# The last stage turned: z stationary, token weights moving, and x turned by VectorE and DMAs instead of TensorE

## The chip, the cores and the metric

One core of a Trainium2 chip runs the whole kernel. The metric is the device time of one execution in microseconds, the median of several runs. Granted TensorE clock in the profile is a share of full speed.

## What is computed

Three blocks in a row, for 4 batches of 768 tokens with 384 channels. The first is a gated linear recurrence over 8 heads, the second four attention experts of which each token takes two, the third mixes tokens and then channels. The change lies in the third:

```python
def _moe2_ref(x, w_theta, w_tok_r, w_tok_i, w_ch):
    theta = x @ w_theta
    cos_t, sin_t = (np.cos(theta), np.sin(theta))
    zr = x * cos_t
    zi = x * sin_t
    yr = np.einsum('ts,bsd->btd', w_tok_r, zr)
    yi = np.einsum('ts,bsd->btd', w_tok_i, zi)
    y = yr + yi
    u = x + y
    return (u + np.maximum(u @ w_ch, 0.0)).astype(np.float32)
```

## The kernel before

Every engine has its own program, written out by hand in the order in which it runs, and semaphores tie them. Four passes of a first stage (recurrence, then experts) fill OT, the experts' weighted outputs of all batches. Then the last stage runs over the batches b = 0 to 3, and within a batch over six tiles s of 128 tokens:

- experts_out(b, s) on TensorE makes x and theta of tile s in two PSUM banks (6 and 7). ScalarE copies x to x2 (keep_x2, L626). VectorE folds theta into one turn (fold: fold_first L967 and L969, fold_rest L976 and L979). ScalarE makes sine and cosine (waves, L631 to L634). GpSimd multiplies them by x (L524, in batch 0 L502). ScalarE rounds the product to z_h (z_hi, L639), VectorE subtracts the rest into z_l (z_lo, by the helper at L952).
- mix(s, t) on TensorE adds what tile s gives to each of six token tiles t, in PSUM banks 0 to 5: 128 tokens by 384 channels each. A product in split precision is three matmuls (split_mm, L1253 to L1255), and there are two weights, so a mix is six matmuls, with a piece of the token weights wt_h or wt_l stationary and z moving.
- During mixing of the last tile (s = 5) the channels begin: VectorE adds x to the bank (add_x, L1227), TensorE turns the sum u by three 128x128 transposes (turn_u, L1563), ScalarE rounds it to uT_h (L843), VectorE makes uT_l (L952), TensorE multiplies by w_ch (channels, nine matmuls), VectorE adds the positive part to u (add_relu, L1211), and SP sends the tile out (L421).

In the profile's names digits are left out: x is x2, z_h stands beside wt_h whichever is stationary. In a row of TensorE the operand named first is the moving one. In batch 0 GpSimd also makes wt_l (L496) between its products.

The next batch is started inside the present one: experts_out(it + 1, 0) runs ahead of mixing of tile 5, experts_out(it + 1, 1) behind it, and the first mixing matmul of the next batch waits for z_lo(it + 1, 0), which stands on VectorE behind the last add_relu. SP carries all DMAs on one queue.

The order of TensorE around the end of a batch:

```python
                for t in range(NT):
                    mix(NT - 1, t)
                    if t >= 1:
                        turn_u(t - 1)
                    if t >= 2:
                        channels(t - 2)
```

Of the kernel before, what the change touches and what calls it, by code (L numbers as in the profile page):

```python
# [22 lines left out]
P = 128  # L23
# [136 lines left out]

SLOW = 6
# [29 lines left out]
def build(nc, fT, qT, kT, vT, v, wq, wk, wv, w_gate, wo, woT, w_theta, w_tok, w_ch, out):  # L191
    with ExitStack() as ctx:
# [112 lines left out]
        uT_h = sb("uT_h", [P, 2, D], F32R)  # L305
        uT_l = sb("uT_l", [P, 2, D], F32R)
# [44 lines left out]
        mix_done, u_done, ut_done, uth_done, utl_done = sem("mix_done"), sem("u_done"), sem("ut_done"), sem("uth_done"), sem("utl_done")  # L351
        ch_done, y_ready, x2_free = sem("ch_done"), sem("y_ready"), [sem(f"x2_free{n}") for n in range(NT)]
# [14 lines left out]
        def _(sp):  # L367
# [54 lines left out]
            for n in range(NT):  # L422
                sp.wait_ge(x2_free[n], 16 * (B + 1))
# [105 lines left out]
        def _(act):  # L529
# [93 lines left out]
            def keep_x2(b, s):  # L623
                act.wait_ge(wo_done, upto(b, NT, s + 1))
                act.wait_ge(x2_free[s], upto(b, 16, 16))
                nc.scalar.copy(x2[:, s, :], ps(out_banks(b, s)[0])[:, 0:D]).then_inc(x2_copied, 1)  # L626
# [38 lines left out]
            for it in range(B):  # L665
# [65 lines left out]
                for n in [*range(RING_X), *range(FIRST_QK, RING)]:  # L731
                    if n == FIRST_QK:
                        if it > B - 2:
                            for t in range(NT):
                                act.sem_inc(x2_free[t], 16)
# [87 lines left out]
            for it in range(B):  # L823
# [33 lines left out]
        def _(dve):  # L857
# [350 lines left out]
            def add_relu(b, t):  # L1208

                dve.wait_ge(ch_done, upto(b, NT, t + 1))  # L1210
                nc.vector.scalar_tensor_tensor(out=x2[:, t, :], in0=ps(t)[:, 0:D], scalar=0.0, in1=x2[:, t, :],  # L1211
                                               op0=ALU.max, op1=ALU.add).then_inc(y_ready, 1)

            for it in range(B):
                for s in range(NT - 1):
# [8 lines left out]
                def add_x(t):  # L1224

                    dve.wait_ge(mix_done, upto(it, NT, t + 1))
                    nc.vector.tensor_tensor(x2[:, t, :], ps(t)[:, 0:D], x2[:, t, :], ALU.add).then_inc(u_done, 1)  # L1227
# [16 lines left out]
                add_relu(it, NT - 1)  # L1244
# [5 lines left out]
        def _(pe):  # L1250
# [40 lines left out]
            def mix(s, t):  # L1291
                at = slice(t * P, (t + 1) * P)
# [266 lines left out]
            for it in range(B):  # L1559
                def turn_u(t):  # L1560
                    pe.wait_ge(u_done, upto(it, NT, t + 1))
                    for c in range(NC):
                        mm = nc.tensor.transpose(ps(t)[:, c * P:(c + 1) * P], x2[:, t, c * P:(c + 1) * P],  # L1563
                                                 ident[:, :])
                    mm.then_inc(ut_done, 1)

                def channels(t):
                    pe.wait_ge(utl_done, upto(it, NT, t + 1))
                    for c in range(NC):
                        at = slice(c * P, (c + 1) * P)  # L1570
                        mm = split_mm(ps(t)[:, 0:D], uT_h[:, t % 2, at], uT_l[:, t % 2, at], wch_h[:, c, :],
                                      wch_l[:, c, :], c == 0, c == NC - 1)
                    mm.then_inc(ch_done, 1)

                for s in range(0 if it >= 1 else 1, NT - 1):
# [7 lines left out]
                    for t in range(NT):  # L1583
                        mix(s, t)
# [9 lines left out]
                for t in range(NT):  # L1594
                    mix(NT - 1, t)
                    if t >= 1:
                        turn_u(t - 1)
# [40 lines left out]
```

## Time and profile before

| | |
|---|---|
| median of 3 runs | 568.41 us (567.17 to 569.14) |
| profiled execution | 567.73 us, its span 566.0 us |
| TensorE, VectorE, ScalarE, GpSimd busy | 95%, 65%, 53%, 23% of the span |
| TensorE clock granted | 0.999 |

The span runs from the first to the last recorded event; the execution's own time has 1.7 us more around it. Busy time is that of instructions alone, and TensorE's overlap each other.

### The profile page before, as it was taken

Reading aid. Unit: us, or ns where it says so; the run is one execution under the profiler, and the core shown is the slowest. Engines: PE = TensorE matmul, PEld = TensorE weight load, DVE = VectorE, ACT = ScalarE, POOL = GpSimd, SP = SyncE. Lnnn points to the kernel's source line nnn. Section 1 sums busy time; section 2 is a strip of 40 time slices with the busy share of each in tenths; the row PEclk is TensorE's granted clock in tenths of the full one; section 3 lists DMA queues with packets and bytes.
Section 4 is the critical chain, followed back from the end, with each engine's and each line's share of the span. In section 5 each row is a group of like instructions: output and inputs, shape, how many; then the busy total and the mean of one; then the engine's idle time right before and its main releaser. Section 6 shows DMA issues by size and latency. Waiting matters only on the chain.

```text
span 566.0 us, 14104 instructions
## 1 busy us (share of the span) xinstructions
PE 537.9 (95%) x5996; PEld 507.5 (90%) x5996; DVE 370.4 (65%) x672; ACT 298.0 (53%) x599; POOL 132.1 (23%) x88
## 2 busy tenths in 40 slices
PE   0999999999999999999999999999999999999997
PEld 0789888898789997899977899999999999999997
DVE  2987887888888777865867677555236544562434
ACT  5759687665876558633578574224222433133311
POOL 2004055044510035100123357112211212022200
PEclk9999999999999999999999999999999999999999
DMA  8948003062210530004500000010001100020002
GB/s 288 345 132 307 2 29 86 3 238 79 78 31 3 182 128 2 1 3 136 203 1 2 1 1 2 0 57 30 0 1 43 42 1 1 14 71 1 1 1 83
DMA packets 17969, 37.24 MB, mean 66 GB/s; under 512 B 2160, under 2 KB 10608, under 8 KB 17392
## 3 DMA queue, kind: packets, MB, share of 16 engines
q1 hardware_dynamic: 17904, 36.32, 18.5%
q8 instruction: 47, 0.77, 0.6%
q14 instruction: 18, 0.15, 0.1%
HBM read 31.46 MB, written 4.72 MB: 64 GB/s over the span
## 4 chain that ended last, share of the span: by engine, by line
PE 78%; ACT 8%; DVE 7%; issue 2%; DMA 2%; POOL 1%; SPq 1%; DVEq 0%; POOLq 0%
PE bank L1253 18%; PE bank L1254 18%; PE bank L1255 18%; ACT prob L728 5%; PE bank L1400 4%; PE bank L1271 4%; PE bank L1463 4%; PE bank L1352 3%; PE bank L1316 3%; PE bank L1359 2%; PE bank L1339 2%; DMA OT<-w_theta 2%; ACT probT L769 1%; PE bank L1563 1%; DVE gate L875 1%
## 5 line engine op out<-in xcount | busy, mean ns | idle before, releaser
L1253 PE MATMUL bank<-z_h,wt_h 128*128 128x384 f32 x288 | 97.7, 339 | 0.0
L1254 PE MATMUL bank<-z_l,wt_h 128*128 128x384 f32 x288 | 97.4, 338 | 0.0
L1255 PE MATMUL bank<-z_h,wt_l 128*128 128x384 f32 x288 | 96.5, 335 | 0.0
L728 ACT ACTIVATE prob<-bank,nmax 128x384 f32<-128x384 f32 (+5 forms) x96 | 60.2, 637 | 20.7 <-DVE nmax L1121 20.7
L524 POOL TENSOR_TENSOR trig<-trig,x 128x768 f32<-128x768 f32 x18 | 33.5, 1864 | 149.5 <-ACT trig L634 92.6
L1121 DVE TENSOR_REDUCE nmax<-bank 128x1 f32<-128x384 f32 (+5 forms) x96 | 54.9, 616 | 9.9 <-PE bank L1406 5.2
L967 DVE TENSOR_SCALAR turns<-bank 128x384 int32<-128x384 f32 x22 | 12.2, 556 | 74.0 <-PE bank L1255 74.0
L1253 PEld LDWEIGHTS bank<-z_h,wt_h 128*128 128x128 f32 x288 | 54.0, 188 | 0.6 <-issue 0.3
L1254 PEld LDWEIGHTS bank<-z_l,wt_h 128*128 128x128 f32 x288 | 54.1, 188 | 0.0
L1255 PEld LDWEIGHTS bank<-z_h,wt_l 128*128 128x128 f32 x288 | 54.0, 188 | 0.0
L843 ACT CAST uT_h<-bank 128x384 fp32r<-128x384 f32 x24 | 11.5, 478 | 78.5 <-PE bank L1563 78.5
L1463 PE MATMUL bank<-probT,Vm 128*64 128x128 f32 x672 | 42.0, 276 | 0.8 <-DVE probT L1141 0.2
L1463 PEld LDWEIGHTS bank<-probT,Vm 128*64 128x64 f32 x672 | 36.2, 137 | 2.9 <-DVE probT L1141 1.4
L626 ACT COPY x<-bank 128x384 f32<-128x384 f32 x24 | 11.5, 481 | 49.7 <-PE bank L1255 44.5
L1352 PE MATMUL bank<-V,probT 128*64 128x48 f32 x768 | 36.0, 220 | 1.0 <-ACT xn L681 0.7
L1007 DVE TENSOR_TENSOR probT<-bank,keep 128x1024 f32<-128x1024 f32 x24 | 29.3, 1221 | 11.7 <-PE bank L1271 11.6
L1400 PE MATMUL bank<-qk_h 64*128 64x512 f32 (+3 forms) x128 | 26.2, 406 | 7.1 <-ACT prob L728 5.4
L1253 PE MATMUL bank<-xT_h,wqk_h 128*128 128x384 f32 x96 | 32.9, 343 | 0.0
L1352 PEld LDWEIGHTS bank<-V,probT 128*64 128x64 f32 x768 | 31.3, 138 | 1.5 <-issue 1.2
L1254 PE MATMUL bank<-xT_l,wqk_h 128*128 128x384 f32 x96 | 32.4, 338 | 0.0
L1255 PE MATMUL bank<-xT_h,wqk_l 128*128 128x384 f32 x96 | 32.4, 337 | 0.0
L1141 DVE COPY probT<-bank 128x896 f32<-128x896 f32 x24 | 26.0, 1085 | 7.8 <-PE bank L1316 7.8
(177 smaller groups left out, 1397.7 us busy)
## 6 DMA issues: line engine op xcount, KB each, us to landing
V<-v SPq DMA_DIRECT2D x4, 1152.0 KB, 10.9
gate<-fT SPq DMA_DIRECT2D x12, 384.0 KB, 3.2
q<-qT SPq DMA_DIRECT2D x12, 384.0 KB, 5.8
k<-kT SPq DMA_DIRECT2D x12, 384.0 KB, 6.3
wt_raw<-w_tok SPq DMA_DIRECT2D x6, 768.0 KB, 8.4
out<-x SPq DMA_DIRECT2D x24, 192.0 KB, 1.9
gate<-fT SPq DMA_DIRECT2D x3, 512.0 KB, 4.8
q<-qT SPq DMA_DIRECT2D x3, 512.0 KB, 9.9
```

Of the source, the lines that this page charges most:

```text
L524: nc.gpsimd.tensor_tensor(trig[:, s % 2, :, :], trig[:, s % 2, :, :], x2[:, s:s + 1, :].broadcast_to([P, 2, D]), ALU.mult).then_inc(z_made, 1)
L728: nc.scalar.activation(prob[:, m % 2, r, at], bank[r][:, at], ACT.Exp, bias=nmax[:, m, k:k + 1], accum_out=den[:, m // 2, which, e:e + 1]) ...
L1007: nc.vector.tensor_tensor(Am[:, c % 2, :, :], bank[c % 2][:, :].rearrange("p (h t) -> p h t", h=H), keep[:, None, :].broadcast_to([P, H, P ...
L1121: nc.vector.tensor_reduce(nmax[:, m, k:k + 1], bank[r][:, columns_of(m, which)], X, ALU.max, negate=True).then_inc(max_done, 1)
L1141: nc.vector.tensor_copy(probT[:, m % 2, 1, :].rearrange("p (c h q) -> p h c q", h=2, q=64), turned(m, 1)).then_inc(pt_copied[0], 1)
L1253: nc.tensor.matmul(o, a_h, b_h, start=start, stop=False)
L1254: nc.tensor.matmul(o, a_h, b_l, start=False, stop=False)
L1255: return nc.tensor.matmul(o, a_l, b_h, start=False, stop=stop)
L1271: mm = nc.tensor.matmul(bank[c % 2][:, slot(h):slot(h) + P], k[r:r + 64, h // 2, at], q[r:r + 64, h // 2, at], start=True, stop=True)
L1352: mm = nc.tensor.matmul(ps(out_bank(c))[own, h * HD:(h + 1) * HD], Am[:, c % 2, slot(h) // P, own], V[:, c, h * HD:(h + 1) * HD], start=c ...
L1400: mm = nc.tensor.matmul(bank[r][:, lo_:hi_], x[rows, a, queries], y[rows, 2 + a, keys], start=fresh_bank and n == 0, stop=False, skip_grou ...
L1463: mm = nc.tensor.matmul(ps(values_bank(m))[64 * r:64 * r + 64, at], Vm[:, s, e * ED:(e + 1) * ED], probT[:, m % 2, r, n * P:(n + 1) * P], ...
```

## The change

- Mixing gives its output turned. A piece of z (128 tokens by 128 channels) is stationary and 384 tokens of the token weights move, so that a bank v holds 128 channels (chunk c) by 384 tokens (one half). There are six such groups v, two halves of three chunks (group_of).
- Channels then need no transposes: w_ch is stationary, uT moves. turn_u is gone. Channels start when mixing of all groups is over.
- x must be turned instead, to be added. VectorE's block transpose turns each 32x32 block of x2 into xb (turn_blocks), and when all six tiles of a batch are there, SP moves blocks from partitions 32i to partitions 32j by 16 SBUF-to-SBUF DMAs into uT. The first add_x of a batch waits for them (x_turned).
- Tokens stand in another order (the host permutes w_tok's columns and orders the output back), and the output is written turned, 192 KB a group as before.
- x2 is no longer the output buffer: keep_x2 waits for the last batch's products and block transposes instead of for output DMAs. VectorE's and ScalarE's order at the end of a batch is new, and uT_h and uT_l hold all groups.

```diff
@@ sync
-            with sp.Fori(0, B) as it:
-                for t in range(NT):
-                    sp.wait_ge(y_ready, upto(it, NT, t + 1))
-                    sp.dma_start(out[it, t], x2[:, t, :]).then_inc(x2_free[t], 16)
...
+            for it in range(B):
+                sp.wait_ge(blocks_turned, upto(it, NT, NT))
+                if it >= 1:
+                    sp.wait_ge(out_done, it * 16 * NT)
+                for i in range(QUARTERS):
+                    for j in range(QUARTERS):
+                        sp.dma_start(uT[j * Q:(j + 1) * Q, :, i * NT * Q:(i + 1) * NT * Q],
+                                     xb[i * Q:(i + 1) * Q, j, :, :]).then_inc(x_turned, 16)
+                for g in range(NT):
+                    c, tokens = group_of(g)
+                    sp.wait_ge(y_ready, upto(it, NT, g + 1))
+                    sp.dma_start(out[it, g], uT[:, c, tokens]).then_inc(out_done, 16)
@@ scalar
-                for t in range(NT):
-                    act.wait_ge(ut_done, upto(it, NT, t + 1))
-                    if t >= 2:
-                        act.wait_ge(ch_done, upto(it, NT, t - 1))
-                    nc.scalar.copy(uT_h[:, t % 2, :], ps(t)[:, 0:D]).then_inc(uth_done, 1)
+                for v in range(NT):
+                    c, tokens = group_of(v)
+                    act.wait_ge(u_done, upto(it, NT, v + 1))
+                    nc.scalar.copy(uT_h[:, c, tokens], uT[:, c, tokens]).then_inc(uth_done, 1)
                     if it < B - 1:
-                        if t == 0:
+                        if v == 2:
+                            keep_x2(it + 1, 0)
+                        if v == 3:
                             act.wait_ge(zl_done, upto(it, NT, NT))
                             waves(it + 1, 0)
-                        if t == 3:
-                            keep_x2(it + 1, 0)
-                        if t == 5:
+                        if v == 5:
@@ vector
+            def turn_blocks(b, s):
+
+                dve.wait_ge(x2_copied, upto(b, NT, s + 1))
+                if b >= 1:
+                    dve.wait_ge(ch_done, upto(b - 1, NT, NT))
+                nc.vector.transpose(xb[:, :, :, s * Q:(s + 1) * Q].rearrange("p j c t -> p c j t"),
+                                    x2[:, s, :].rearrange("p (c j t) -> p c j t", c=NC, j=QUARTERS)
+                                    ).then_inc(blocks_turned, 1)
...
                     z_lo(it, s + 1)
+                    if s == 0:
+                        turn_blocks(it, 0)
+                        turn_blocks(it, 1)
+                    elif s == 1:
+                        turn_blocks(it, 2)
+                    if 1 <= s < NT - 2:
+                        turn_blocks(it, s + 2)
...
+                    dve.wait_ge(mix_done, upto(it, NT, v + 1))
+                    if v == 0:
+                        dve.wait_ge(x_turned, (it + 1) * 16 * QUARTERS * QUARTERS)
+                    nc.vector.tensor_tensor(uT[:, c, tokens], ps(v)[:, 0:HALF], uT[:, c, tokens], ALU.add).then_inc(u_done, 1)
...
                 add_x(0)
-                if it < B - 1:
-                    fold_rest(it + 1, 0)
-                for t in range(NT):
-                    if t + 1 < NT:
-                        add_x(t + 1)
-                    dve.wait_ge(uth_done, upto(it, NT, t + 1))
-                    lo(uT_l[:, t % 2, :], ps(t)[:, 0:D], uT_h[:, t % 2, :], utl_done)
-                    if t == NT - 1:
-                        if it < B - 1:
-                            fold(it + 1, 1)
-                    if t >= 1:
-                        add_relu(it, t - 1)
-                add_relu(it, NT - 1)
+                for v in range(1, NT):
+                    add_x(v)
+                    u_lo(v - 1)
+                    if v == NC and it < B - 1:
+                        fold_rest(it + 1, 0)
+                u_lo(NT - 1)
+                for v in range(NT):
+                    add_relu(it, v)
+                    if v == NC - 1 and it < B - 1:
+                        fold(it + 1, 1)
                 if it < B - 1:
                     z_lo(it + 1, 0)
@@ tensor
-                    mm = split_mm(ps(t)[:, 0:D], wt_h[:, n * NT + s, at], wt_l[:, n * NT + s, at],
-                                  z_h[:, s, n, :], z_l[:, s, n, :], s == 0 and n == 0, s == NT - 1 and n == 1)
+                    mm = split_mm(ps(v)[:, 0:HALF], z_h[:, s, n, rows], z_l[:, s, n, rows], wt_h[:, n * NT + s, tokens],
+                                  wt_l[:, n * NT + s, tokens], s == 0 and n == 0, s == NT - 1 and n == 1)
...
+                    if v % NC == 0:
+                        pe.wait_ge(utl_done, upto(it, NT, v + NC))
...
-                for t in range(NT):
-                    mix(NT - 1, t)
-                    if t >= 1:
-                        turn_u(t - 1)
-                    if t >= 2:
-                        channels(t - 2)
+                for v in range(NT):
+                    mix(NT - 1, v)
                 if it < B - 1:
                     banks_read(it + 1, 1)
                     experts_out(it + 1, 1)
-                turn_u(NT - 1)
-                channels(NT - 2)
-                channels(NT - 1)
+                for v in range(NT):
+                    channels(v)
```

VectorE at the end of a batch, before. The first rows are the last channel tiles (x<-bank,x is add_x at L1227 and add_relu at L1211), then the fold of the next batch's tile 1, the last two add_relu and z_l of its tile 0:

```order
L1227 TENSOR_TENSOR x<-bank,x 128x384
L952 TENSOR_TENSOR uT_l<-bank,uT_h 128x384
L1211 SCALAR_TENSOR_TENSOR x<-bank,x 128x384
L952 TENSOR_TENSOR uT_l<-bank,uT_h 128x384
L967 TENSOR_SCALAR turns<-bank 128x384
L969 SCALAR_TENSOR_TENSOR r<-turns,bank 128x384
L976 SCALAR_TENSOR_TENSOR r<-turns,r 128x384
L979 TENSOR_SCALAR r<-r 128x384
L1211 SCALAR_TENSOR_TENSOR x<-bank,x 128x384 x2
L952 TENSOR_TENSOR z_l<-trig,z_h 128x768
```

The same place in the changed kernel (L1272 is add_x, L1237 add_relu, L977 the subtraction, L992 to L1004 the fold):

```order
L1272 TENSOR_TENSOR uT<-bank,uT 128x384
L977 TENSOR_TENSOR uT_l<-uT,uT_h 128x384 x2
L1237 SCALAR_TENSOR_TENSOR uT<-bank,uT 128x384 x3
L992 TENSOR_SCALAR turns<-bank 128x384
L994 SCALAR_TENSOR_TENSOR r<-turns,bank 128x384
L1001 SCALAR_TENSOR_TENSOR r<-turns,r 128x384
L1004 TENSOR_SCALAR r<-r 128x384
L1237 SCALAR_TENSOR_TENSOR uT<-bank,uT 128x384 x3
L977 TENSOR_TENSOR z_l<-trig,z_h 128x768
```

The fold moved from behind the last uT_l to behind the third add_relu, and three add_relu stand between it and z_l instead of two.

SP's queue of the last stage in the changed kernel, from the first batch on:

```order
L443 DMA uT<-xb 32x3x192 [waits blocks_turned]
L443 DMA uT<-xb 32x3x192 x15
L448 DMA out<-uT 128x384 [waits y_ready] x6
L443 DMA uT<-xb 32x3x192 [waits out_done,blocks_turned]
L443 DMA uT<-xb 32x3x192 x15
```

Before, only the output DMAs stood there; now 16 block transfers stand ahead of the six outputs of each batch.

## Rows read from the trace of the kernel before

**Rows 1.** The page, busy us by engine (share of the span) and instructions.

```profile
PE 537.9 (95%) x5996; PEld 507.5 (90%) x5996; DVE 370.4 (65%) x672; ACT 298.0 (53%) x599; POOL 132.1 (23%) x88
```

**Rows 2.** Windows: the last stage, its length, then busy us (instructions) by engine.

```profile
core 0: us, PE busy (x) PEld busy (x) DVE busy (x) ACT busy (x) POOL busy (x), PEclk, DMA share, GB/s
320.00:566.00 246.00, 242.92 (x1435) 241.20 (x1432) 121.78 (x189) 81.63 (x147) 55.44 (x29) 1.00 0.06 20
```

**Rows 3.** Instructions grouped by line: busy us, mean ns, then idle time before.

```profile
L1253 PE MATMUL bank<-z_h,wt_h 128*128 128x384 f32 x288 | 97.7, 339 | 0.0
...
L1563 PE MATMUL bank<-ident,x 128*128 128x128 f32 x72 | 11.7, 271 | 0.0
```

**Rows 4.** The chain of waits, batch 3: start us, us, what.

```profile
547.24 0.33 PE bank L1563 x3
```

**Rows 5.** Timeline of TensorE: start us, us, engine, line, operation.

```profile
381.51 0.33 PE L1253 MATMUL bank<-wx_h,OT_h 128*128 128x384 f32 x1
...
383.59 0.36 PE L1253 MATMUL bank<-z_h,wt_h 128*128 128x384 f32 x1
...
423.43 0.33 PE L1253 MATMUL bank<-z_h,wt_h 128*128 128x384 f32 x1
...
424.48 0.34 PE L1253 MATMUL bank<-z_h,wt_h 128*128 128x384 f32 x1
...
445.36 0.39 PE L1253 MATMUL bank<-z_h,wt_h 128*128 128x384 f32 x1
...
507.23 0.37 PE L1253 MATMUL bank<-z_h,wt_h 128*128 128x384 f32 x1
```

**Rows 6.** Timeline of VectorE in batch 3 (in brackets: idle before, what ended it).

```profile
532.66 0.56 DVE L967 TENSOR_SCALAR turns<-bank 128x384 int32<-128x384 f32 x1 [5.38 <-PE bank L1255]
...
534.72 0.95 DVE L952 TENSOR_TENSOR z_l<-trig,z_h 128x768 fp32r<-128x768 f32 x1
...
546.23 0.56 DVE L1227 TENSOR_TENSOR x<-bank,x 128x384 f32<-128x384 f32 x1 [6.11 <-PE bank L1255]
```

**Rows 7.** Timeline of VectorE, TensorE and GpSimd in batch 0.

```profile
330.47 0.56 DVE L967 TENSOR_SCALAR turns<-bank 128x384 int32<-128x384 f32 x1 [1.18 <-PE bank L1255]
...
335.61 2.60 DVE L952 TENSOR_TENSOR z_l<-trig,z_h 128x768 fp32r<-128x768 f32 x1
...
338.58 0.33 PE L1253 MATMUL bank<-z_h,wt_h 128*128 128x384 f32 x1
...
339.89 3.98 POOL L496 TENSOR_TENSOR wt_l<-wt_raw,wt_h 128x768 fp32r<-128x768 f32 x2
...
340.02 2.14 DVE L976 SCALAR_TENSOR_TENSOR r<-turns,r 128x384 f32<-128x384 int32 x1
...
351.62 0.94 DVE L952 TENSOR_TENSOR z_l<-trig,z_h 128x768 fp32r<-128x768 f32 x1
...
362.88 0.55 DVE L1227 TENSOR_TENSOR x<-bank,x 128x384 f32<-128x384 f32 x1
```

**Rows 8.** DMA issues: KB each and us to landing; issue times; landing of identh's DMAs.

```profile
out<-x SPq DMA_DIRECT2D x24, 192.0 KB, 1.9
...
382.29 0.91 SPq L421 DMA_DIRECT2D out<-x  x2
...
L402 SPq DMA_DIRECT2D identh<-identb x4: 536/596/597, 19.5 to 23.2; - x4
...
DMA to landing us min/median/max: 4.3/5.4/6.5
```

**Rows 9.** Timeline of VectorE and GpSimd at the handover from batch 0 to 1.

```profile
381.30 0.36 DVE L979 TENSOR_SCALAR r<-r 128x384 f32<-128x384 f32 x1
...
382.51 0.94 DVE L952 TENSOR_TENSOR z_l<-trig,z_h 128x768 fp32r<-128x768 f32 x1
...
383.22 1.96 POOL L524 TENSOR_TENSOR trig<-trig,x 128x768 f32<-128x768 f32 x1 [8.79 <-ACT trig L634]
```

**Rows 10.** Timeline of TensorE and VectorE at the end of the program.

```profile
562.58 0.34 PE L1255 MATMUL bank<-wch_h,uT_l 128*128 128x384 f32 x1
...
562.96 0.56 DVE L1211 SCALAR_TENSOR_TENSOR x<-bank,x 128x384 f32<-128x384 f32 x1 [1.01 <-PE bank L1255]
```

More of the change, by code:

```diff
@@ L158, in banks_shared, with group_of @@
     return columns_of(m, 1).stop > 512
+QUARTERS = 4
+Q = P // QUARTERS
+def group_of(v):
+    half, c = divmod(v, NC)
+    return c, slice(half * HALF, (half + 1) * HALF)
 SLOW = 6
@@ L304, in build @@
         trig = sb("trig", [P, 2, 2, D])
-        uT_h = sb("uT_h", [P, 2, D], F32R)
-        uT_l = sb("uT_l", [P, 2, D], F32R)
+        uT = sb("uT", [P, NC, T])
+        blocks_ctx = ExitStack()
+        xb = sb("xb", [P, QUARTERS, NC, NT * Q], where=blocks_ctx)
+        blocks_ctx.close()
+        uT_h = sb("uT_h", [P, NC, T], F32R)
+        uT_l = sb("uT_l", [P, NC, T], F32R)
         after_Am = probT[:, :, :, :].rearrange("p b r n -> p (b r n)")[:, 2 * H * P:2 * H * P + 3 * D]
@@ L350, in build @@
         absd, trig_done, z_made, zh_done, zl_done = sem("absd"), sem("trig_done"), sem("z_made"), sem("zh_done"), sem("zl_done")
-        mix_done, u_done, ut_done, uth_done, utl_done = sem("mix_done"), sem("u_done"), sem("ut_done"), sem("uth_done"), sem("utl_done")
-        ch_done, y_ready, x2_free = sem("ch_done"), sem("y_ready"), [sem(f"x2_free{n}") for n in range(NT)]
+        mix_done, u_done, uth_done, utl_done = sem("mix_done"), sem("u_done"), sem("uth_done"), sem("utl_done")
+        ch_done, y_ready, out_done = sem("ch_done"), sem("y_ready"), sem("out_done")
+        blocks_turned, x_turned = sem("blocks_turned"), sem("x_turned")
         W_QK, W_O, W_OTH, W_CH, W_TH, W_OT = 0, 1536, 2304, 3072, 4224, 5376
@@ L1222, in _, with add_x, u_lo @@
                             split_outputs(it + 1)
-                def add_x(t):
-                    dve.wait_ge(mix_done, upto(it, NT, t + 1))
-                    nc.vector.tensor_tensor(x2[:, t, :], ps(t)[:, 0:D], x2[:, t, :], ALU.add).then_inc(u_done, 1)
+                def add_x(v):
+                    c, tokens = group_of(v)
+                    dve.wait_ge(mix_done, upto(it, NT, v + 1))
+                    if v == 0:
+                        dve.wait_ge(x_turned, (it + 1) * 16 * QUARTERS * QUARTERS)
+                    nc.vector.tensor_tensor(uT[:, c, tokens], ps(v)[:, 0:HALF], uT[:, c, tokens], ALU.add).then_inc(u_done, 1)
+                def u_lo(v):
+                    c, tokens = group_of(v)
+                    dve.wait_ge(uth_done, upto(it, NT, v + 1))
+                    lo(uT_l[:, c, tokens], uT[:, c, tokens], uT_h[:, c, tokens], utl_done)
                 if it < B - 1:
@@ L1559, in _, with channels @@
             for it in range(B):
[L1560 to L1572, printed above, removed]
+                def channels(v):
+                    c, tokens = group_of(v)
+                    if v % NC == 0:
+                        pe.wait_ge(utl_done, upto(it, NT, v + NC))
+                    rows = slice(c * P, (c + 1) * P)
+                    for d in range(NC):
+                        mm = split_mm(ps(v)[:, 0:HALF], wch_h[:, d, rows], wch_l[:, d, rows], uT_h[:, d, tokens],
+                                      uT_l[:, d, tokens], d == 0, d == NC - 1)
                     mm.then_inc(ch_done, 1)
@@ L1582, in _ @@
                         pe.wait_ge(tok_lo, 2 * s + 2)
-                    for t in range(NT):
-                        mix(s, t)
+                    for v in range(NT):
+                        mix(s, v)
                 if it < 1:
@@ L1602, in _ @@
                     experts_out(it + 1, 1)
-                turn_u(NT - 1)
-                channels(NT - 2)
-                channels(NT - 1)
+                for v in range(NT):
+                    channels(v)
 def kernel(**inputs):
@@ L1627 @@
         "w_theta": rows(inputs["moe2_w_theta"]),
-        "w_tok": rows(np.concatenate([inputs["moe2_w_tok_r"].T, inputs["moe2_w_tok_i"].T])),
+        "w_tok": rows(np.concatenate([inputs["moe2_w_tok_r"].T, inputs["moe2_w_tok_i"].T])
+                      .reshape(2 * T, NT, QUARTERS, Q).transpose(0, 2, 1, 3).reshape(2 * T, T)),
         "w_ch": rows(inputs["moe2_w_ch"]),
@@ L1631 @@
     arrays = {n: np.ascontiguousarray(a) for n, a in arrays.items()}
-    nc = bacc.Bacc("TRN2", target_bir_lowering=False, num_devices=1)
+    nc = bacc.Bacc("TRN2", target_bir_lowering=False, num_devices=1, dynamic_dma_scratch_size=8192)
     args = [nc.dram_tensor(n, a.shape, F32, kind="ExternalInput").ap() for n, a in arrays.items()]
-    args.append(nc.dram_tensor("out", (B, NT, P, D), F32, kind="ExternalOutput").ap())
+    args.append(nc.dram_tensor("out", (B, NT, P, HALF), F32, kind="ExternalOutput").ap())
     build(nc, *args)
     r = run_bass_kernel_spmd(nc, [arrays], core_ids=[0])
-    return r.results[0]["out"].reshape(B, T, D)
+    y = r.results[0]["out"].reshape(B, 2, NC, P, QUARTERS // 2, NT, Q)
+    return np.ascontiguousarray(y.transpose(0, 5, 1, 4, 6, 2, 3).reshape(B, T, D))
```

21 lines of the change are left out of this document (11 added, 10 removed).

## The prediction, made before the changed kernel ran

> **What bounds the kernel now.** I began with the page: TensorE is busy 95% of the span, VectorE 65%, ScalarE 53% [rows 1]. The windows show where that is tightest: from 320 us to the end, the last stage, TensorE works 242.9 of 246 us at full granted clock, VectorE 121.8 [rows 2]. In this stage work taken off TensorE is time, as long as nobody else becomes late, so the reader should look for two things: what a TensorE item costs in the stream, and how much room the others have. The grouped lines name the items: 864 mixing matmuls (L1253, and L1254 and L1255 with as many) and the 72 transposes of L1563 [rows 3]. Their mean durations overlap each other and are no price. The price is in the chain of waits, where three transposes together stand for 0.33 us [rows 4]. As a check, the first mixing matmuls of batches 1, 2 and 3 start 61.77 and 61.87 us apart; a batch has 216 mixing, 72 output and 54 channel matmuls, 342 at 0.175 us (six of them lie between 423.43 and 424.48 us), some 59.7 us [rows 5]. Six groups of transposes hold the other 2.1 to 2.2 us, 0.36 us each.
>
> **The change, part by part.**
>
> *TensorE.* It loses 24 groups of three transposes: 24 x 0.36 = **8.6 us off**, all of it on the path. The number of matmuls and their 384 moving columns stay, but in mixing and channels what stands still and what moves is exchanged. The matmuls of the experts' outputs, with other operands in these places, go at 0.173 us (twelve from 381.51 to 383.59) against 0.1745 [rows 5], so the exchange of 216 + 54 matmuls in four batches is worth 1080 x 0.0015 = 1.6 us less, or as much more. I take 0, because both sizes stay.
>
> *VectorE, turning x.* 24 block transposes of 128x384 are added, six a batch, each behind a z_l. No row has this operation. Below stands the quiet 128x384 operation of 0.36 us [rows 9], above the 128x768 subtraction of 0.95 us [rows 6]; I take 0.56, as other 128x384 operations here [rows 6]. That is 3.4 us a batch on an engine that works half of this stage [rows 2], and costs nothing unless it makes the fold behind it late. In batches 1 to 3 that fold waits for TensorE anyway (5.38 us, [rows 6]). Batch 0 is the narrow place: GpSimd splits token weights, z_l took 2.60 us instead of 0.95 and ended at 338.21, and mixing of tile 2 began at 338.58 [rows 7]. But the two transposes ahead of it fill the idle 1.18 us before 330.47, and of the two at 338.2 the second ends at 339.3, 0.45 us after the fold began before; that fold's third operation stands still until GpSimd's instruction is over at 341.9 in any case (2.14 us for 0.56, [rows 7]). I take 0.
>
> That stretching the Trainium skill explains (SBUF — State Buffer, the port pair shared by VectorE and GpSimd): an operation with two SBUF inputs waits for a whole GpSimd instruction that started first. The trace agrees, with those 2.60 us [rows 7]. By the same page a transpose with one input would stay out of it; no row here shows that.
>
> *Block transfers.* Each batch adds 16 DMAs on SP's queue, 72 KB each, SBUF to SBUF. They start when the sixth block transpose is done, and all must have landed before VectorE's first addition of x (L1227 before). Batch 0: z_l of tile 4 ends at 352.56, its transpose at 353.1, and the addition began at 362.88 [rows 7]. Batch 3: 534.72 + 0.95 + 0.56 = 536.2 and 546.23 [rows 6]; batches 1 and 2 have twelve matmuls more in between, 2.1 us. A late addition does not stop TensorE at once. Mixing of tile 5 began 1.25 us before the addition (five matmuls and 0.38 us, [rows 5, 10]), call that M. In batches 0 to 2 the outputs of the next batch's tile 1, wanted 36 matmuls after M, wait for keep_x2, which now stands behind the third uT_h: from the landing two additions, a uT_l, an addition, uT_h and the copy, 4 x 0.56 + 1.1 = 3.3 us. So landing may take until M + 3.0, 364.6 in batch 0. In batch 3 the channels want three uT_l at M + 6.3, seven operations behind the landing, 3.9 us: until 547.4. The rooms are **11.5, 13.8, 13.8 and 11.1 us**. The need: two output DMAs were issued in 0.91 us, 0.46 each, and such a 192 KB landed 1.9 us after issue [rows 8]: 15 x 0.46 + 1.9 = **8.8 us**. The upper bound: of eight SBUF-to-SBUF DMAs of 16 KB, some 0.62 us apart (four of them and what lies between start from 19.5 to 23.2 us), the slowest landed in 6.5 us, with long loads ahead of them [rows 8]: 15 x 0.62 + 6.5 = 15.8 us. I stay by 8.8, since SP's queue is empty here, and take **0 us**, with 2.3 us to spare at the narrowest.
>
> *The order at the end of a batch.* Channels start only when mixing is over, groups 0 to 2 after three uT_l and 3 to 5 after six. VectorE needs 1.11 us a group, mixing 1.05, so three are ready at M + 5.7 and wanted at M + 6.3 (batch 3) or M + 8.4; six are ready by M + 11 and wanted 4.7 us after the first three. Free. The handover is not. The fold of the next batch's tile 1 goes out after the third add_relu instead of after the last uT_l. Count from the start of channels: the third add_relu ends at 4.71 + 0.21 + 0.56 = 5.5 us, the fold 2.1 us later [rows 6] at 7.6; GpSimd's product starts 1.56 us after a fold's end (381.66 to 383.22, [rows 9]), at 9.1, and holds its 1.9 us till 11.0. z_l of the next batch's tile 0 is ready at 10.1, behind the last add_relu, and must wait for it; before, z_l began at 382.51, ahead of GpSimd [rows 9]. It ends at 11.0 + 0.9 = 11.9, and mixing, due at 9.4 + 2.1 = 11.5, starts 0.45 us late. Three handovers: **1.3 us on**. The bounds are 0, if z_l gets there first, and 1.9 us each, a whole GpSimd instruction.
>
> *Rest.* The end of the program is as before, a last matmul, add_relu 0.38 us behind its start, one output DMA [rows 10]: 0. keep_x2 waits for things long over instead of for the output's landing, and SP's loop is written out: 0.
>
> Sum: -8.6 + 1.3 = -7.3 us. The profiled execution took 567.73 us (span 566.0), so 560.4; it stands 0.7 us under the median of the three runs, 568.41, for which I say **561.1 us**.
>
> **Rivals.**
>
> *The blocks land late (0.12).* For it: 16 issues in a row on one queue, each on only 32 partitions, and the bound of 15.8 us. Against: 0.46 us an issue. If a batch's transfers take X us, the stalls above all four rooms are 4X - 50.2; at X = 14.4 they eat the gain, and every us more costs 4. At the bound they are 13.0 us, which makes **574.1 us, slower than before**. With X between 11 and 14.4 the time is 561 to 568.
>
> *One landing after another (0.03).* If each landing were paid in full, 16 x 1.9 = 30.4 us a batch, 4 x 30.4 - 50.2 = 71.4 us more: 632 us. Against: the eight small DMAs went out 0.62 us apart and took 4.3 to 6.5 us, so they overlapped [rows 8].
>
> The Trainium skill (DMA: Bandwidth & Descriptors, anatomy of one DMA) gives a fixed cost of about 2.0 us a transfer, mostly completion; the 1.9 us of rows 8 agree, and as an estimate from that page alone 16 in a row would be 32 us a batch. Its page VectorE: DVE Perf Modes (rules for kernel authors) would keep a 128x128 transpose on TensorE where PSUM will do, which speaks against this change.
>
> *VectorE crowded in batch 0 (0.08).* If the block transposes wait for GpSimd as z_l did, some 1.9 us each, their two pairs push folds back by 2.6 and 3.2 us, against 0.4 us of room at tile 2 [rows 7]: 2 to 5 us of stall, 564.5 us.
>
> *The exchange helps, or the handover costs nothing (0.07).* Matmuls at 0.173 us give 559.5 us, no wait for GpSimd 559.8, most of both 558.8.
>
> **How the numbers follow.** The forecast has 0.70, and the time is its: 561.1 us. The range 558.8 to 566.5 us holds it, the last rival, the crowded batch and the mild part of the late blocks; out are the bad part of these and the serial case. Within 0.3% of 568.4, 1.7 us, is about what a measurement of this kernel cannot tell from no change. Faster: 0.70 + 0.07 + 0.07 (crowded, but not fully) + 0.02 = 0.86. Slower: 0.03 + half of 0.12 = 0.09. Same: the 0.05 left.
>
> **What would show it.** Right: no transposes on TensorE after 324 us, batches about 60.1 us apart, transfers landed before the first addition, a z_l of 1.7 us or more at each handover with TensorE idle some 0.4 us there. Wrong: the first addition released by a DMA later than the rooms above, with TensorE idle behind it; block transposes of over 1 us; matmuls of the last stage off 0.175 us.

## The result, and the profile after

The changed kernel takes **560.51 us** (median of 4 runs, 560.09 to 561.22) against 568.20 us for the kernel before (4 runs, 567.17 to 569.14): a ratio of 0.9869, 95% interval 0.9852 to 0.9886. The prediction was 561.1 us, in a range of 558.8 to 566.5. The profiled execution took 560.85 us, its span is 559.1 us, 6.9 us less than before.

The page after, busy line and chain, with the group of mixing matmuls and the two kinds of DMA of the last stage:

```profile
PE 530.0 (95%) x5924; PEld 499.0 (89%) x5924; DVE 384.8 (69%) x696; ACT 298.7 (53%) x599; POOL 131.9 (24%) x88
...
PE 71%; DVE 11%; ACT 7%; SPq 4%; issue 3%; DMA 2%; POOL 0%; DVEq 0%; POOLq 0%
...
L1301 PE MATMUL bank<-wt_h,z_h 128*128 128x384 f32 x288 | 97.3, 338 | 0.4
...
uT<-xb SPq DMA_DIRECT2D x64, 72.0 KB, 2.1
out<-uT SPq DMA_DIRECT2D x24, 192.0 KB, 1.9
```

TensorE still bounds it, and its matmuls last what they did in [rows 3] (338 ns in the mean, 339 before); the 72 transposes are gone. New in the chain is SPq, SP's queue: the block transfers now stand on the path for a stretch. Where that is can be read from the waits between 320 and 560 us (engine, operation and line that waits, who let it go: us in total, times, longest):

```profile
DVE uT L1272 <- DMA uT<-xb: 12.1, 4, 7.9
...
PEld bank L1301 <- DVE z_l L977: 1.4, 3, 0.5
PEld bank L1301 <- ACT x L654: 1.1, 1, 1.1
...
PEld bank L1301 <- DVE uT_l L977: 0.6, 1, 0.6
```

VectorE waits for the transfers in all four batches. TensorE waits in five places: at three handovers for z_l, and once each for keep_x2 (L654) and for uT_l. The first are the term of +1.3 us of the prediction; the other two it had put at 0. Their places, in order of time (start, duration, engine, line, operation; in brackets the idle time ahead of it and who ended it):

```profile
337.33 2.57 POOL L528 TENSOR_TENSOR trig<-trig,x 128x768 f32<-128x768 f32 x1
...
338.11 1.02 DVE L1245 STREAM_TRANSPOSE xb<-x 128x384 f32<-128x384 f32 x2
...
353.02 10.89 SPq L443 DMA_DIRECT2D uT<-xb  x16
...
362.24 0.55 DVE L994 SCALAR_TENSOR_TENSOR r<-turns,bank 128x384 f32<-128x384 int32 x1
365.52 1.02 DVE L1272 TENSOR_TENSOR uT<-bank,uT 128x384 f32<-128x384 f32 x2 [2.73 <-DMA uT<-xb]
...
367.52 0.34 PE L1303 MATMUL bank<-wt_h,z_l 128*128 128x384 f32 x1
368.66 0.44 PE L1301 MATMUL bank<-wx_h,OT_h 128*128 128x384 f32 x1 [0.80 <-ACT x L654]
...
379.88 1.84 POOL L550 TENSOR_TENSOR trig<-trig,x 128x768 f32<-128x768 f32 x1 [6.47 <-ACT trig L662]
...
380.89 1.65 DVE L977 TENSOR_TENSOR z_l<-trig,z_h 128x768 fp32r<-128x768 f32 x1
...
382.59 0.44 PE L1301 MATMUL bank<-wt_h,z_h 128*128 128x384 f32 x1
...
442.43 0.44 PE L1301 MATMUL bank<-wt_h,z_h 128*128 128x384 f32 x1
...
502.24 0.44 PE L1301 MATMUL bank<-wt_h,z_h 128*128 128x384 f32 x1
...
531.16 10.22 SPq L443 DMA_DIRECT2D uT<-xb  x16
...
542.99 1.02 DVE L1272 TENSOR_TENSOR uT<-bank,uT 128x384 f32<-128x384 f32 x2 [7.87 <-DMA uT<-xb]
...
545.98 0.34 PE L1303 MATMUL bank<-wt_h,z_l 128*128 128x384 f32 x1
546.60 0.45 PE L1301 MATMUL bank<-uT_h,wch_h 128*128 128x384 f32 x1 [0.28 <-DVE uT_l L977]
```

**The transfers.** In batch 0 the addition (L1272) begins 12.5 us after the first issue, in batch 3 11.8 us; the prediction had rooms of 11.5 and 11.1 us for it, and so it was 1.0 and 0.7 us late. TensorE's next matmul starts 1.14 and 0.62 us behind the last one, instead of 0.17: 0.97 and 0.45 us are lost. (The brackets say 0.80 and 0.28, since they count from the end of the last matmul; below, a wait of TensorE is counted from start to start, less 0.17, unless it is called idle.) In batches 1 and 2, with 2 us more room, nothing is.

**The handover** from batch 0 to 1 is the rows from 379.88 to 382.59 us. GpSimd's product, released by the fold that now comes early, starts 1.0 us ahead of z_l, which takes 1.65 us instead of 0.95. The first mixing matmuls of batches 1 to 3 are 59.84 and 59.81 us apart, 61.77 and 61.87 before [rows 5].

### The profile page after: what moved, and what is told of

Same layout as the page of the kernel before. It is cut to its first block, busy times and chain, and to the rows that moved or that the text cites. A ratio compares the mean times of both kernels' runs of the same rounds, so it can differ in the third digit from the quotient of the medians.

```text
span 559.1 us, 13960 instructions
## 1 busy us (share of the span) xinstructions
PE 530.0 (95%) x5924; PEld 499.0 (89%) x5924; DVE 384.8 (69%) x696; ACT 298.7 (53%) x599; POOL 131.9 (24%) x88
## 4 chain that ended last, share of the span: by engine, by line
PE 71%; DVE 11%; ACT 7%; SPq 4%; issue 3%; DMA 2%; POOL 0%; DVEq 0%; POOLq 0%
PE bank L1301 16%; PE bank L1303 15%; PE bank L1302 15%; ACT prob L756 5%; PE bank L1512 5%; PE bank L1319 4%; PE bank L1449 4%; PE bank L1401 3%; SPq L443 3%; PE bank L1365 3%; PE bank L1408 2%; PE bank L1388 2%; DMA OT<-w_theta 2%; DVE gate L900 1%; DVE nmax L1146 1%
## 5 line engine op out<-in xcount | busy, mean ns | idle before, releaser
L1301 PE MATMUL bank<-wt_h,z_h 128*128 128x384 f32 x288 | 97.3, 338 | 0.4
L1303 PE MATMUL bank<-wt_h,z_l 128*128 128x384 f32 x288 | 96.7, 336 | 0.0
L1302 PE MATMUL bank<-wt_l,z_h 128*128 128x384 f32 x288 | 96.5, 335 | 0.0
L992 DVE TENSOR_SCALAR turns<-bank 128x384 int32<-128x384 f32 x22 | 12.2, 554 | 64.7 <-PE bank L1303 64.6
L1301 PEld LDWEIGHTS bank<-wt_h,z_h 128*128 128x128 f32 x288 | 54.0, 188 | 1.7 <-DVE z_l L977 1.4
L1303 PEld LDWEIGHTS bank<-wt_h,z_l 128*128 128x128 f32 x288 | 54.1, 188 | 0.0
L1302 PEld LDWEIGHTS bank<-wt_l,z_h 128*128 128x128 f32 x288 | 54.0, 187 | 0.0
L654 ACT COPY x<-bank 128x384 f32<-128x384 f32 x24 | 11.5, 480 | 56.7 <-PE bank L1303 56.7
L868 ACT CAST uT_h<-uT 128x384 fp32r<-128x384 f32 x24 | 11.8, 511 | 44.6 <-DVE uT L1272 44.4
L659 ACT ACTIVATE trig<-r 128x384 f32<-128x384 f32 x22 | 11.6, 527 | 38.9 <-DVE r L1004 38.9
```

The source lines that it names most:

```text
L1301: nc.tensor.matmul(o, a_h, b_h, start=start, stop=False)
L1302: nc.tensor.matmul(o, a_h, b_l, start=False, stop=False)
L1303: return nc.tensor.matmul(o, a_l, b_h, start=False, stop=stop)
```

## The experiments

The first stage is the same in all these kernels, yet the last stage (VectorE's first turn of a tile's angles, L992, L967 before the change) began between 325.58 and 328.12 us in the profiled executions. So I compare, besides the medians, the **length of the last stage**, from that start to the end of the span: 239.7 us before, 232.8 after. Line numbers shift by a few where lines were added.

### The transfers in whole rows

A transfer writes 32 partitions, 3 runs of 768 bytes on each. Here uT is ordered so that it is one run of 2304 bytes. The outputs, read from the same uT, now go out in two runs of 768 bytes a partition instead of one of 1536.

```diff
-        uT = sb("uT", [P, NC, T])
+        uT = sb("uT", [P, QUARTERS, NC, NT * Q])
...
-                        sp.dma_start(uT[j * Q:(j + 1) * Q, :, i * NT * Q:(i + 1) * NT * Q],
+                        sp.dma_start(uT[j * Q:(j + 1) * Q, i, :, :],
...
-                    sp.dma_start(out[it, g], uT[:, c, tokens]).then_inc(out_done, 16)
+                    sp.dma_start(split(out[it, g]), uT_of(g)).then_inc(out_done, 16)
```

> uT is laid out by token quarter first, so that a block transfer writes one run of 2304 bytes in each of 32 partitions (32 runs a DMA instead of 96); everything else stays. In the changed kernel a transfer takes 0.60 us to issue, 0.64 us apart, and the sixteenth lands 11.8 us after the first was issued (15 x 0.64 + 2.1), which leaves TensorE waiting 1.1 us in batch 0 and 0.9 us in batch 3. Theory A (an issue is priced by its runs): 0.45 us or less an issue, 9 us or less in all, both waits gone, 2.0 us less than the changed kernel, 558.5 us. Theory B (an issue between SBUF and SBUF has a fixed price, as the 64-run DMAs of identh at 0.60 us say): 0.60 us again, 560.5 us.

Measured: 560.73 us (560.45 to 563.39), ratio 0.9876 (0.9849 to 0.9902), last stage 232.7 us. The 16 transfers of batch 0, and the addition behind them (its line is now L1279):

```profile
353.02 10.40 SPq L450 DMA_DIRECT2D uT<-xb  x16
...
364.98 1.02 DVE L1279 TENSOR_TENSOR uT<-bank,uT 128x384 f32<-128x384 f32 x2 [2.25 <-DMA uT<-xb]
```

10.40 instead of 10.89 us, and the addition 12.0 us after the first issue instead of 12.5. With a third of the runs the median issue of a transfer went only from 599 to 591 ns (507 to 1523 here, 591 to 1344 without the edit): fewer runs in what it writes do not make it cheap. The last stage is the same within 0.1 us, but not because nothing changed. TensorE's two waits fell from 0.97 and 0.45 us to 0.49 and 0.30, and its last matmul starts 229.1 us into the stage instead of 229.6. Against that, an output in two runs took 0.53 us to issue and 2.3 us to land, instead of 0.33 and 1.9, so that the time from the last add_relu to the end of the span grew from 2.3 to 2.7 us. The form of a transfer does enter the price of its issue; by what rule, this run does not show.

### The transfers on two queues

Ten stay on SP's queue and six go out from ScalarE.

```diff
+BLOCKS = [(i, j) for i in range(QUARTERS) for j in range(QUARTERS)]
+ON_SP = 10
...
-                for i in range(QUARTERS):
-                    for j in range(QUARTERS):
+                for i, j in BLOCKS[:ON_SP]:
...
+                act.wait_ge(blocks_turned, upto(it, NT, NT))
+                if it >= 1:
+                    act.wait_ge(out_done, it * 16 * NT)
+                for i, j in BLOCKS[ON_SP:]:
+                    act.dma_start(uT[j * Q:(j + 1) * Q, :, i * NT * Q:(i + 1) * NT * Q],
+                                  xb[i * Q:(i + 1) * Q, j, :, :]).then_inc(x_turned, 16)
```

> Six of the sixteen block transfers of a batch are issued by ScalarE, behind its last z_hi, ten stay with SP. If late landing costs the changed kernel 2.0 us (1.1 in batch 0, 0.9 in batch 3): in batch 0 SP's ten land at 353.0 + 9 x 0.64 + 2.1 = 360.9 and ScalarE's six by 361.5, ahead of the first addition; both waits are gone, 558.5 us. If the transfers themselves share something scarce and two queues only interleave, the landing stays at 12 us and the time at 560.5 us. If ScalarE's issues delay its own work more than that, over 560.5.

Measured: 560.0 us (559.23 to 561.38), ratio 0.9858 (0.9832 to 0.9885), last stage 231.3 us. Batch 0:

```profile
353.09 7.19 SPq L446 DMA_DIRECT2D uT<-xb  x10
...
355.22 4.10 ACTq L872 DMA_DIRECT2D uT<-xb  x6
...
362.75 0.55 DVE L1281 TENSOR_TENSOR uT<-bank,uT 128x384 f32<-128x384 f32 x1
```

The addition follows the fold without a wait, and of TensorE's waits in the last stage only the three for z_l are left. The last stage is 1.5 us shorter, about as much as the two waits that are gone (0.97 + 0.45). The late transfers cost 1.5 us. The median is only 0.5 us lower, less than the runs of one kernel differ; the trace carries this reading.

### The fold ahead of all additions of the positive part

```diff
                 u_lo(NT - 1)
+                if it < B - 1:
+                    fold(it + 1, 1)
                 for v in range(NT):
                     add_relu(it, v)
-                    if v == NC - 1 and it < B - 1:
-                        fold(it + 1, 1)
```

> The fold of the next batch's tile 1 goes out right behind the last uT_l, ahead of all six add_relu, as the kernel before had it. Theory of the handover: GpSimd's product then runs some 3 to 5 us earlier and is over when z_l of tile 0 is ready; z_l takes 0.95 us instead of 1.65, TensorE's three waits of about 0.45 us go: 1.4 us less than the changed kernel, 559.1 us. Rival: add_relu 1 to 3 come 2 us later and the last one too, z_l moves with it, and nothing is won: 560.5 us or more.

Measured: 559.86 us (559.1 to 562.01), ratio 0.9861 (0.9836 to 0.9887), last stage 231.5 us. The same handover:

```profile
377.49 1.85 POOL L550 TENSOR_TENSOR trig<-trig,x 128x768 f32<-128x768 f32 x1 [4.48 <-ACT trig L662]
...
380.49 0.95 DVE L977 TENSOR_TENSOR z_l<-trig,z_h 128x768 fp32r<-128x768 f32 x1
...
381.90 0.33 PE L1301 MATMUL bank<-wt_h,z_h 128*128 128x384 f32 x1
...
441.30 0.33 PE L1301 MATMUL bank<-wt_h,z_h 128*128 128x384 f32 x1
...
500.70 0.33 PE L1301 MATMUL bank<-wt_h,z_h 128*128 128x384 f32 x1
```

The product is over 1.15 us before z_l begins, z_l takes its quiet 0.95 us, and the batches are 59.40 us apart, 0.44 and 0.41 less. Three handovers are 1.3 us, all that the last stage lost (the median fell by 0.65 us, within the spread of the runs). So z_l was late because it ran beside GpSimd, and that came from where the fold stood.

### Both edits together

```diff
+                for i, j in BLOCKS[:ON_SP]:
...
+                for i, j in BLOCKS[ON_SP:]:
...
+                if it < B - 1:
+                    fold(it + 1, 1)
                 for v in range(NT):
                     add_relu(it, v)
```

> Both repairs together: the fold ahead of the add_relus (alone it took the span from 559.1 to 557.4 us) and six block transfers on ScalarE's queue (alone 557.6). If the two waits are separate, as the theory says (landing in batches 0 and 3, z_l at the three handovers), they add: span 559.1 - 1.7 - 1.5 = 555.9, some 557.5 us, faster than both kernels. If one hides the other: 559 us or more.

Measured: **558.5 us** (557.49 to 559.87), ratio 0.9838 (0.9812 to 0.9864), last stage 229.9 us. TensorE has no wait left in the last stage. This is 2.9 us under the changed kernel's 232.8, about the sum of the two edits (1.5 + 1.3), and it is the best version found: all five runs lie below the four of the changed kernel (560.09 us and more), though the intervals of the two ratios overlap (0.9812 to 0.9864 and 0.9852 to 0.9886).

### The transposes put back

Three transposes of the identity go ahead of each group of channels. Their result isn't used.

```diff
                     for d in range(NC):
+                        nc.tensor.transpose(ps(v)[:, d * P:(d + 1) * P], ident[:, :], ident[:, :])
+                    for d in range(NC):
                         mm = split_mm(ps(v)[:, 0:HALF], wch_h[:, d, rows], wch_l[:, d, rows], uT_h[:, d, tokens],
```

> Three 128x128 transposes of the identity (into the bank that the group's channels then overwrite; they are not used) are put ahead of each group's channels: 24 groups, 72 transposes, TensorE's removed work alone put back. If a group costs the 0.36 us taken from the batches' distances: +8.6 us over the changed kernel, 569.1 us; by the chain's 0.33 us +7.9, 568.4. Rival: if the gain came from elsewhere (the exchange of operands, fewer waits), less than +5 us. Part may fall into waits that exist already (0.45 us at three handovers is behind them and stays, the 0.9 us of batch 3 stays too).

Measured: 568.77 us (567.62 to 569.98, 12 runs), ratio 1.0013 (0.9999 to 1.0028), last stage 240.3 us. The whole gain is gone. The first mixing matmuls of batches 1 to 3, and the second group of transposes in batch 3, between channel matmuls that otherwise start 0.173 us apart:

```profile
383.64 0.33 PE L1301 MATMUL bank<-wt_h,z_h 128*128 128x384 f32 x1
...
445.16 0.33 PE L1301 MATMUL bank<-wt_h,z_h 128*128 128x384 f32 x1
...
506.68 0.33 PE L1301 MATMUL bank<-wt_h,z_h 128*128 128x384 f32 x1
...
553.12 0.34 PE L1303 MATMUL bank<-uT_h,wch_l 128*128 128x384 f32 x1
553.29 0.49 PE L1615 MATMUL bank<-ident 128*128 128x128 f32 x3
553.54 0.42 PE L1301 MATMUL bank<-uT_h,wch_h 128*128 128x384 f32 x1
553.80 0.33 PE L1302 MATMUL bank<-uT_l,wch_h 128*128 128x384 f32 x1
```

Channels are longer here, so z_l has the time it needs: it takes 0.95 us and TensorE doesn't wait for it. The batches are 61.52 us apart both times. Against the version with the fold moved, which has no wait at the handover either (59.40), that is 2.12 us a batch and 0.353 us a group: 24 groups are **8.5 us**, where the prediction had 8.6. The last stage grew by less, 7.5 us, since the 1.3 us of the handovers went, while the two waits for the transfers grew by 0.3 us in sum (0.87 us each).

### Block transposes done twice

```diff
+                nc.vector.transpose(xb[:, :, :, s * Q:(s + 1) * Q].rearrange("p j c t -> p c j t"),
+                                    x2[:, s, :].rearrange("p (c j t) -> p c j t", c=NC, j=QUARTERS)
+                                    ).then_inc(once_turned, 1)
+                dve.wait_ge(once_turned, upto(b, NT, s + 1))
```

> Each block transpose on VectorE is made twice, 24 more of 0.57 us. Theory (they lie in VectorE's idle time, and in batch 0 ahead of operations that wait for GpSimd anyway): only the sixth one's doubling counts, since the transfers start behind it, 0.6 us later in batch 0 and in batch 3: +1.1 us over the changed kernel, 561.6 us. Rival (VectorE is crowded in batch 0): the folds come late, TensorE waits for z_l of tiles 2 to 4, +2 to +5 us, 562.5 to 565.5 us.

Measured: 562.91 us (561.67 to 564.01), ratio 0.9902 (0.9873 to 0.993), last stage 234.2 us, 1.4 more than after. The two of each pair took 0.56 and 0.58 us in the mean, and TensorE waits for none of the folds behind them; what grew are the two waits known from above:

```profile
371.15 0.44 PE L1305 MATMUL bank<-wx_h,OT_h 128*128 128x384 f32 x1 [1.45 <-ACT x L654]
...
549.77 0.44 PE L1305 MATMUL bank<-uT_h,wch_h 128*128 128x384 f32 x1 [0.89 <-DVE uT_l L977]
```

0.65 and 0.61 us more, one operation each: the transfers start when the last block transpose is done, and that one now comes an operation later. The 24 added ones cost 1.3 us, and only by way of the transfers; the 24 of the change cost nothing by crowding VectorE, whose folds TensorE never waits for. The median rose by 2.4 us, more than the last stage did; in the profiled execution that stage had begun 1.85 us later than in the changed kernel's. Why the first stage took longer there isn't settled; the edit doesn't touch it.

### The transfers made later

Four of them go out twice, and SP waits for these to land before it issues the sixteen, so that the last lands some 4 us later.

```diff
+                for j in range(QUARTERS):
+                    sp.dma_start(uT[j * Q:(j + 1) * Q, :, 0:NT * Q], xb[0:Q, j, :, :]).then_inc(x_turned, 16)
+                sp.wait_ge(x_turned, 16 * (it * (QUARTERS + 1) * QUARTERS + QUARTERS))
...
-                        dve.wait_ge(x_turned, (it + 1) * 16 * QUARTERS * QUARTERS)
+                        dve.wait_ge(x_turned, (it + 1) * 16 * (QUARTERS + 1) * QUARTERS)
```

> Ahead of the sixteen block transfers of a batch four of them are made once more and SP waits till they have landed: 3 x 0.64 + 2.1 + 0.1 = 4.1 us, so that the last landing comes 15.9 us after the first issue (16.6 in batch 0, whose first issue is longer) instead of 11.8 (12.5). By the rooms of 11.5, 13.8, 13.8 and 11.3 us TensorE waits 5.1, 2.1, 2.1 and 4.6 us, 13.9 in all instead of 1.5: +12.4 us over the changed kernel, 572.9 us, slower than the kernel before. Rival: if the waits are not set by the landing, or the rooms of batches 1 and 2 are larger, +8 us or less.

Measured: 579.74 us (579.43 to 580.33), ratio 1.0207 (1.018 to 1.0234), last stage 252.1 us. TensorE is idle for 4.87, 1.79, 2.99 and 4.33 us. Counted from start to start, as the expectation was, its waits are 5.04, 1.96, 3.16 and 4.50 us, 14.7 in sum, where 5.1, 2.1, 2.1 and 4.6, 13.9 in sum, were expected; the third is a microsecond longer because the sixteen transfers of batch 2 took 11.41 us to issue instead of 10.21. But the last stage is 19.3 us longer than after, not 12.4. Windows around the waits (length, then busy time and count of PE, PEld, DVE, ACT and POOL, granted clock, DMA share, GB/s), and matmuls behind the first:

```profile
366.00:376.00 10.00, 5.13 (x20) 4.81 (x19) 6.10 (x13) 4.64 (x10) 0.79 (x1) 0.70 0.15 33
...
370.00:371.00 1.00, 0.00 (x0) 0.00 (x0) 0.89 (x3) 0.75 (x2) 0.00 (x0) 0.50 0.00 0
...
430.00:440.00 10.00, 8.21 (x47) 7.89 (x46) 6.13 (x13) 4.72 (x11) 0.81 (x1) 1.00 0.14 30
492.00:502.00 10.00, 7.01 (x35) 6.70 (x34) 5.61 (x12) 3.62 (x8) 0.00 (x0) 0.88 0.21 45
```

```profile
372.32 0.69 PE L1304 MATMUL bank<-wx_h,OT_h 128*128 128x384 f32 x1 [4.87 <-ACT x L657]
372.80 0.52 PE L1305 MATMUL bank<-wx_l,OT_h 128*128 128x384 f32 x1
373.12 0.52 PE L1306 MATMUL bank<-wx_h,OT_l 128*128 128x384 f32 x1
...
376.32 0.52 PE L1304 MATMUL bank<-uT_h,wch_h 128*128 128x384 f32 x1
...
376.89 0.33 PE L1306 MATMUL bank<-uT_h,wch_l 128*128 128x384 f32 x1
377.07 0.34 PE L1304 MATMUL bank<-uT_h,wch_h 128*128 128x384 f32 x1
```

After 4.87 us of idling TensorE's matmuls last 0.52 us and start 0.32 us apart, and the granted clock of the window is 0.70 of full; it is at 0.50, the level of 1.2 GHz, from 370 us on, while TensorE still waits. From 376.9 us on the matmuls are back at 0.33 and 0.174. The window with the wait of 1.79 us keeps its 1.00, the one with 2.99 us has 0.88. Slow steps stand behind three of the waits, 14, 12 and 14 of them (most of 0.32 us), no such series elsewhere in the stage; together they are 6.0 us longer than steps of 0.174. With 14.66 - 1.42 = 13.2 us of added waits that accounts for 19.2 of the 19.3 us. So the rooms of the rival "blocks land late" were right, and its price was too low: with the addition 15.9 to 17.1 us after the first issue this run took 579.7 us, where the rival had 574.1 us for 15.8.

### Weights still, z moving

Mixing has z moving and a piece of the token weights stationary again, everything else as in the change. The sums are then no longer those of the product, so this kernel shows only what the exchange costs in time.

```diff
-                    mm = split_mm(ps(v)[:, 0:HALF], z_h[:, s, n, rows], z_l[:, s, n, rows], wt_h[:, n * NT + s, tokens],
-                                  wt_l[:, n * NT + s, tokens], s == 0 and n == 0, s == NT - 1 and n == 1)
+                    at = slice(v * P, (v + 1) * P)
+                    mm = split_mm(ps(v)[:, 0:HALF], wt_h[:, n * NT + s, at], wt_l[:, n * NT + s, at],
+                                  z_h[:, s, n, :], z_l[:, s, n, :], s == 0 and n == 0, s == NT - 1 and n == 1)
```

> In mixing alone the operands are put back: a piece of the token weights stationary, 384 channels of z moving (the sums in the banks are then those of the untransposed product, so the output is not the reference's); all else as in the changed kernel. The sum of the parts measured so far leaves 1.2 us that the exchange must have given (mixing matmuls 0.1738 us apart instead of 0.1745). Theory: 0.1745 us again, +0.6 to +1.2 us, 561.1 to 561.7 us. Rival: no difference by operand, 560.5 us, and the 1.2 us come from elsewhere.

Measured: 561.38 us (560.78 to 562.68), ratio 0.9878 (0.9852 to 0.9905), last stage 233.5 us, 0.6 more than after. The first mixing matmuls of batches 1 to 3:

```profile
383.91 0.45 PE L1301 MATMUL bank<-z_h,wt_h 128*128 128x384 f32 x1
...
443.96 0.44 PE L1301 MATMUL bank<-z_h,wt_h 128*128 128x384 f32 x1
...
503.98 0.45 PE L1301 MATMUL bank<-z_h,wt_h 128*128 128x384 f32 x1
```

They are 60.05 and 60.02 us apart, 0.21 us a batch more than in the changed kernel, with the same wait at the handover: 0.8 us in four batches. The last stage grew by only 0.6 us because the longer mixing leaves the transfers more time: their two waits are 0.83 and 0.35 us instead of 0.97 and 0.45. The steps from one mixing matmul to the next show the same. In the timeline of 394 to 420 us, a stretch without a wait, some 125 of them take 0.1735 us on average in the changed kernel, 0.1747 in this one and 0.1748 in the kernel before; the 22 steps between output matmuls there take 0.1736 in all three. The exchange helps a little, on its own. Channels gain nothing by it; before, their last ten stand 0.173 us apart, as all do now.

## Why the prediction was right

| term, us | predicted | measured | by |
|---|---|---|---|
| 24 groups of transposes | -8.6 | -8.5 | transposes put back |
| z_l behind GpSimd at three handovers | +1.3 | +1.3 | fold moved |
| transfers late | 0 | +1.5 | two queues |
| exchange of operands | 0 (+-1.6) | -0.8 | weights still |
| block transposes on VectorE | 0 | 0 | done twice |
| end of the program | 0 | -0.2 | the two traces |
| sum | -7.3 | -6.7 | span: -6.9 |

*The transposes* held to a tenth of a microsecond. Their price came from two views that agreed within a tenth, the chain (0.33 us a group, [rows 4]) and the distance of batches against a count of matmuls (0.36, [rows 5]), of which the second was taken; the mean duration of a group [rows 3] would have been no guide.

*The handover* held in size and mechanism: the product starts first, z_l stretches, and TensorE idles (z_l of 1.65 us or more was the sign named). Counted from the start of channels (370.85 us) the product began at 9.0 us and z_l at 10.0, where 9.1 and 10.1 had been worked out. The Trainium skill (SBUF — State Buffer, Who interferes with whom) told it this way, and moving the fold alone took the stretching away, 1.65 to 0.95 us. By the same page an operation with at most one SBUF input stays out, unless it runs in one of VectorE's two-port modes. The trace agrees for the block transposes: the two at 338.11 us lie within GpSimd's product of 337.33 to 339.90 us and stand for 1.02 us together, and all 24 took 0.53 to 0.57 us by the trace's list of them, where I had taken 0.56. One input alone is no safeguard, though: the fold's last operation, which has one, took 0.36 us when quiet (at 369.59 us) and 1.89 us beside GpSimd's wt_l. And the change made one more operation that GpSimd can hold up: uT_l is now made from uT and uT_h, both in SBUF, where it had read a bank, and two of them took 2.37 us together beside GpSimd's product of 371.57 to 373.41 us. TensorE waited for neither, so this cost nothing here.

```profile
339.86 3.96 POOL L522 TENSOR_TENSOR wt_l<-wt_raw,wt_h 128x768 fp32r<-128x768 f32 x2
...
342.15 1.89 DVE L1004 TENSOR_SCALAR r<-r 128x384 f32<-128x384 f32 x1
...
371.92 2.37 DVE L977 TENSOR_TENSOR uT_l<-uT,uT_h 128x384 fp32r<-128x384 f32 x2 [0.58 <-ACT uT_h L868]
```

*The block transfers* are the step that failed: "the need: 15 x 0.46 + 1.9 = 8.8 us" measured 12.5 and 11.8 us. The 0.46 us was half of a row that joins two output DMAs, SBUF to HBM [rows 8]. It is no issue price even of those, which the trace's list has at 0.33 us; each waits for an add_relu of its own. The eight SBUF-to-SBUF DMAs of rows 8 had stood 0.62 us apart, were the nearer kind, and I had used them for the upper bound alone. With 0.62 and 1.9 us the need would have been 11.2 us, just over the narrowest room. The issues stood 0.64 us apart in batch 3 (10.22 us for 16) and 0.68 in batch 0 (10.89), and landing took 2.1: 11.7 and 12.3 us. The rooms themselves (11.5 and 11.1 us) were right to 0.3 us: they give stalls of 1.0 and 0.7, and 0.97 and 0.45 came. The two wider batches lost nothing. So the term put at 0 us, with 2.3 us to spare, measured +1.5 us.

*The exchange* was put at 0 "because both sizes stay", and gave 0.8 us, inside its bounds; channels, which the bound counted too, gained nothing. *The end of the program* was put at 0, and the time from the last add_relu to the end of the span is 2.27 us instead of 2.48. Part of the agreement of the total is thus luck: of terms put at 0, one came as +1.5 and two as -0.8 and -0.2, and two thirds of the miss cancel. Between the sum of the measured terms (-6.7) and the span's -6.9 no run tells. The medians fell by more than the spans, 7.7 us, and the forecast's 0.6 us from the median is within what runs of one kernel differ.

*The rivals.* "Blocks land late" happened in its mild form, 1.5 us, not as the cause of a loss. One landing after another is out: sixteen were over 11.8 to 12.5 us after the first issue, not 30. Each took 2.1 us to land, and the chain of sixteen paid that once. VectorE crowded in batch 0 is out: the pairs of block transposes passed GpSimd, and TensorE waited there for nothing.

## What to carry to other kernels

Where one engine is busy through a stage, an operation taken off it is worth its place in the stream (here 0.35 us for three transposes), to be read from distances between fixed points and not from durations; but list every dependent chain that the replacement opens and compare its length with the room it has. A chain of many DMAs on one queue takes their count times the spacing of issues of that same kind of transfer, plus one landing; take both numbers from the nearest kind that a trace holds, and spread the chain over two queues when the sum comes near its room (here 0.7 and 1.0 us over). And when work for a shared port can be released earlier, look who starts beside it: moving one fold by three operations was worth 1.3 us.

## What was not expected of the hardware

- An SBUF-to-SBUF transfer of 72 KB takes 0.60 us to issue (median of 64; least 0.59), which with a third of the runs stayed at 0.59, and lands 2.1 us later. For 192 KB from SBUF to HBM it was 0.33 and 1.9 us: the smaller transfer costs its queue more. The same 192 KB read in two runs a partition took 0.53 and 2.3 us (whole rows).
- TensorE's granted clock fell behind a wait of 4.87 us, and matmuls stood 0.32 us apart for some 4 us afterwards. A wait of 1.79 us in the same kernel left it at full, and so did the 0.97 us of the changed kernel, whose window from 366 to 376 us shows 1.00. A stall can thus cost nearly half as much again as its length: 13.2 us of added waits made 19.3 us.
- Which operand moves makes 0.001 us a mixing matmul (0.1747 against 0.1735) with the same sizes. Why isn't known.
